# One scores round of batch 2, its keys and its softmax, one position earlier in the first stage

## What is computed

```
B, H, S, D = 8, 8, 576, 64;  pool = 8
k_p, v_p = k, v averaged over groups of 8 keys             # 72 keys
attn = softmax(q @ k_p^T / sqrt(D));  x = attn @ v_p       # 4608 tokens x 512
h = (x @ w1) * (x @ w2) @ w3;  x = h @ w_out               # 512 -> 1024 -> 1024 -> 512
e = argmax(x @ w_gate + modality_bias[modality_id]);  g = softmax(...)[e]
out = g * (relu(x @ w1[e]) @ w2[e])                        # 8 experts, 512 -> 1024 -> 512
```

## Time and profile before

| | |
|---|---|
| Median of 3 runs | 1188.93 us (1187.56 to 1189.38) |
| Profiled execution | 1191.04 us |
| Its span in the trace | 1189.3 us |
| Mean granted clock of PE in it | 0.996 |
| PE busy | 1154.7 us, 97% |
| DVE, ACT, POOL busy | 641.3, 397.3, 404.3 us |

### The profile page before, as it was taken

One profiled execution on the slowest core, in us unless ns is written; L12 is line 12 of the kernel. 1 busy time (PEld: TensorE's weight loads), 2 busy tenths in 40 slices (PEclk: granted clock), 3 DMA queues, 4 the chain that ended last, 5 costly groups with the idle time before them and its releaser, 6 DMA issues.

```text
span 1189.3 us, 29760 instructions
## 1 busy us (share of the span) xinstructions
PE 1154.7 (97%) x12126; PEld 1083.7 (91%) x12127; DVE 641.3 (54%) x1228; ACT 397.3 (33%) x906; POOL 404.3 (34%) x385
## 2 busy tenths in 40 slices
PE   8899989999999999999999999999999999999996
PEld 7678879999999999999999999998998999899895
DVE  0799688898987974753444557622222252222222
ACT  1566455555555541333223224111111141111110
POOL 2355866777766645550000000211211212121111
PEclk9999999999999999999999999999999999999998
DMA  9755362644726414345555555241111101111111
GB/s 349 266 173 149 100 198 78 201 121 148 197 79 200 102 44 125 107 133 140 134 138 135 135 163 176 70 179 45 46 51 35 44 27 55 44 52 45 35 48 41
DMA packets 99890, 137.12 MB, mean 115 GB/s; under 512 B 16835, under 2 KB 66115, under 8 KB 99780
## 3 DMA queue, kind: packets, MB, share of 16 engines
q1 hardware_dynamic: 40340, 78.77, 22.4%
q10 hardware_dynamic: 53040, 36.29, 10.8%
q0 software_dynamic: 6400, 20.50, 5.4%
HBM read 92.99 MB, written 43.06 MB: 114 GB/s over the span
## 4 chain that ended last, share of the span: by engine, by line
PE 55%; DVE 0%; POOL 0%; issue 0%; DMA 0%; ACT 0%; ACTq 0%; POOLq 0%; DVEq 0%
PE ab L728 6%; PE x2p L727 6%; PE ab L727 6%; PE ab L729 6%; PE x2p L729 6%; PE x2p L728 6%; PE rt L728 6%; PE rt L727 6%; PE rt L729 6%; PE sct L916 1%; PE ab L907 0%; DMA out<-y_out,tok_c 0%; DVE gl L1537 0%; POOL gst L635 0%; DVE kb L1511 0%
## 5 line engine op out<-in xcount | busy, mean ns | idle before, releaser
L728 PE MATMUL ab<-xtl,e1h 128*128 128x256 f32 x608 | 170.7, 281 | 0.0
L727 PE MATMUL ab<-xth,e1h 128*128 128x256 f32 x608 | 169.6, 279 | 0.0
L729 PE MATMUL ab<-xth,e1l 128*128 128x256 f32 x608 | 169.3, 278 | 0.0
L1400 ACT ACTIVATE hth<-ab 128x512 fp32r<-128x512 f32 x76 | 45.4, 597 | 333.9 <-PE ab L729 316.7
L707 POOL DMA_INDIRECT out<-y_out,tok_c x38 | 38.4, 1010 | 319.6 <-DVE y_out L2019 319.0
L1998 DVE SCALAR_TENSOR_TENSOR htl<-ab,hth 128x512 fp32r<-128x512 f32 x76 | 52.4, 691 | 156.2 <-ACT hth L1400 151.6
L728 PEld LDWEIGHTS ab<-xtl,e1h 128*128 128x128 f32 x608 | 114.5, 188 | 0.7
L727 PEld LDWEIGHTS ab<-xth,e1h 128*128 128x128 f32 x608 | 114.1, 188 | 1.0 <-issue 0.4
L729 PEld LDWEIGHTS ab<-xth,e1l 128*128 128x128 f32 x608 | 114.3, 188 | 0.0
L1085 ACT ACTIVATE pb<-pb,rc 128x72 f32<-128x72 f32 x320 | 83.2, 347 | 58.9 <-DVE rc L1472 58.9
L727 PE MATMUL ab<-xh,wh 128*128 128x256 f32 x336 | 96.4, 287 | 4.2 <-DVE kb L1511 2.9
(11 more groups left out here) (229 smaller groups left out, 3346.5 us busy)
## 6 DMA issues: line engine op xcount, KB each, us to landing
gr<-g_rows SPq DMA_DIRECT2D x36, 512.0 KB, 4.4
kv<-in_v SPq DMA_DIRECT2D x24, 512.0 KB, 4.9
qt<-in_q ACTq DMA_DIRECT2D x38, 256.0 KB, 3.3
kv<-in_k SPq DMA_DIRECT2D x16, 576.0 KB, 5.4
g_rows<-gst ACTq DMA_DIRECT2D x72, 128.0 KB, 2.8
g_rows<-gst ACTq DMA_DIRECT2D x36, 256.0 KB, 3.3
x_rows<-xr SPq DMA_DIRECT2D x36, 256.0 KB, 4.1
stage<-in_moe_w SPq DMA_DIRECT2D x8, 1024.0 KB, 10.5
```

The lines of the kernel that those rows point to most:

```text
L727: pe.matmul(outp, lh, rh, start=first, stop=False)
L728: pe.matmul(outp, lh, rl, start=False, stop=False)
L729: return pe.matmul(outp, ll, rh, start=False, stop=last)
L1400: act.activation(hth[:, 2 * n:2 * n + 2, :].rearrange("p f n -> p (f n)"), ab[n // 2][:, n % 2, :], ACT.Relu).then_inc(hth_ready, 1)
```

## The change

Round 0 of batch 2 goes on PE from behind product 4 of position 3 to behind product 4 of position 2 of stage 0. Its maximum and subtraction, its sum and inverse (DVE) and its exponential (ACT) go to position 2 as well; its normalising (ACT) goes to the end of position 3, its transpose (DVE) to one place earlier in position 0 of stage 1. POOL pools the keys of batch 2 (both halves) directly behind the second product of position 1 instead of behind the first quarter of position 2. Since the scores now come ahead of the weighing of batch 1, the wait of round 0 for the copied outputs of batch 1 goes, and the weighing waits for the subtraction of round 0 instead, as in the later stages. Nothing is added or taken out.

```diff
--- before.py
+++ after.py
@@ -650,7 +650,7 @@
                     first_quarter(POS * b + i)
                     if i == 0 and b + 1 < B:
                         pool_v(b + 1, 2)
-                    if i == (1 if b else 2) and b + 2 < B:
+                    if b and i == 1 and b + 2 < B:
                         pool_k(b + 2, 0)
                         pool_k(b + 2, 1)
                     if b and i == 2 and b + 2 < B:
@@ -658,6 +658,9 @@
                     if i == 3 and b + 2 < B:
                         pool_v(b + 2, 1)
                     other_quarters(POS * b + i)
+                    if b == 0 and i == 1:
+                        pool_k(2, 0)
+                        pool_k(2, 1)
 
             pool.wait_ge(pv_done, 2 * B)
             pool.memset(ident[:, :], 0.0).then_inc(pool_done, 1)
@@ -790,9 +793,7 @@
                     pe.wait_ge(sub_done, r)
                 if b == 1 and m == 0:
                     pe.wait_ge(xf_ready, 5)
-                if b == 2 and m == 0:
-                    pe.wait_ge(xf_ready, 8 + 5)
-                if b > 2 and m == 0:
+                if b > 1 and m == 0:
                     pe.wait_ge(xf_ready, 8 * (b - 2) + 5)
                 if b and m == 1:
                     pe.wait_ge(xf_ready, 8 * (b - 1) + 5)
@@ -814,7 +815,7 @@
                     pe.wait_ge(vp4_in, 64 * (b + 1))
                     if b == 0:
                         pe.wait_ge(w34_copied, w34_no(FC - 2, 0))
-                    if b > 1 and b + 1 < B:
+                    if b and b + 1 < B:
                         pe.wait_ge(sub_done, AT * (b + 1) + 1)
                 else:
                     pe.wait_ge(xf_ready, 8 * b + 4)
@@ -865,7 +866,7 @@
                         weigh_v(1, 0)
                     if i == 3 and n == 1:
                         weigh_v(1, 1)
-                    if i == 3 and n == 4:
+                    if i == 2 and n == 4:
                         score(2, 0)
 
             def position(b, i):
@@ -1267,6 +1268,7 @@
                     store_g(1, 1)
                     norm(1, 4)
                     store_g(2, 0)
+                    exp_p(2, 0)
                 if i == 3:
                     raw_x(1, 0)
                     copy_p(3, 0)
@@ -1283,7 +1285,7 @@
                 if i == 3:
                     hi_x(1, 4)
                     hi_x(1, 5)
-                    exp_p(2, 0)
+                    norm(2, 0)
 
             def position(b, i):
                 at = POS * b + i
@@ -1295,7 +1297,6 @@
                         exp_p(b + 1, 1)
                     copy_p(at, 1)
                     if b == 1:
-                        norm(2, 0)
                         exp_p(2, 1)
                     store_g(at - 1, 1)
                     if att:
@@ -1730,7 +1731,9 @@
                     u2(2)
                     u3(2)
                     soft_turn(1, 4)
+                    soft_max(2, 0)
                     u4_c22(2)
+                    soft_sum(2, 0)
                 if i == 3:
                     u2(3)
                     x_sum(1, 3)
@@ -1742,7 +1745,6 @@
                     x_sum(1, 5)
                     lo_x(1, 1)
                     lo_x(1, 2)
-                    soft_max(2, 0)
                 c12(i)
                 if i == 3:
                     for n in range(3, 6):
@@ -1760,7 +1762,7 @@
                     u2(at)
                     if b == 1:
                         lo_x(1, 6)
-                        soft_sum(2, 0)
+                        soft_turn(2, 0)
                     u3(at)
                     if b == 1:
                         soft_max(2, 1)
@@ -1768,7 +1770,6 @@
                         soft_max(b + 1, 2)
                     u4_c22(at)
                     if b == 1:
-                        soft_turn(2, 0)
                         soft_sum(2, 1)
                         soft_max(2, 2)
                     if att:
```

## The result

| | before | changed |
|---|---|---|
| Median (22 runs each) | 1187.80 us (1185.84 to 1190.47) | 1190.40 us (1187.66 to 1193.47) |
| Ratio | | 1.0022, 95% interval 1.0015 to 1.0029 |
| Profiled execution, its span | 1191.04, 1189.3 us | 1189.49, 1187.8 us |

The change makes the kernel **slower, by 2.6 us or 0.22%**. I had forecast -0.4 us. The median of 1190.40 us lies inside my range of 1186.6 to 1190.6 us, but by luck: the range was laid round the median of three runs, 1188.93 us, and that of 22 runs is 1187.80. The difference is what failed.

The account below looks back on a forecast made before the run. PE, 97% busy, bounds the kernel, and DVE bounds PE in this stretch. A start 2.50 us later and a run 2.87 us shorter give -0.4 us: 1188.5 us from the 1188.93 median, range 1186.6 to 1190.6.

Parts of the forecast that it names:

- What leaves the run: DVE's gapless run from 131.78 to 156.93 us loses round 0's softmax work, 2.87 us: 22.28 instead of 25.15 us.
- what it costs at the start: PE waits 1.7 us at round 0 for POOL's keys, plus 0.81 us of round: DVE's run starts 2.50 us later.
- The wait for the keys: PE at round 0 of batch 2, near 122.3 us, stands still 1.7 us for the keys pooled by POOL.
- the wait of product 2 of stage 1: PE's wait for DVE there, 1.91 us at 143.50 before, was to fall to about 0.6 us.
- Product 0: First product of stage 1 on PE: at 141.0 instead of 138.5 us, with a wait of over 1 us.
- rival 3: POOL behind position 1: the keys come later still, pooling stretched to 7.85 us; +1.7 us, 1190.6 us; chance 0.07.
- The two x_sums: DVE sums with two SBUF inputs, 1.04 and 1.66 us: waits for POOL shift between them and cancel, taken as 0.
- rival 1: Keys in time at round 0, or DVE pays less to POOL: -2.1 us, 1186.9 us; chance 0.17.
- rival 2: Lock between DVE and POOL falls worse, each x_sum waiting a whole POOL instruction: +0.8 us, 1189.7 us; chance 0.15.
- The signs that I had named for being right: Key wait about 1.7 us; product 2's about 0.6, product 0's over 1; u2 near 134.3 us, round 3 near 156.7.
- The sum: DVE's run ends at 156.56 against 156.93 us, 0.37 us sooner; round 3 and later waits move with it: net -0.4 us.
- SP's loads of values wait for the pooled keys and start some 3 us sooner: Side effect on SP's queue, counted with the other moved work as costing zero.

Follow-up runs that it names:

- loads_wait: Changed kernel with SP's loads of batch 3's keys and spreading of batch 2's values held until round 4's queries landed; 1187.44 us, 0.9999 to the kernel before.
- spread_held: Changed kernel with only the spreading of batch 2's values held until round 4's queries landed; 1188.48 us, 0.9993 to the kernel before.
- before_again: The kernel before, with no edit, profiled a second time; 1188.93 us, ratio 1.0000.

## Why the prediction was wrong, by its own steps

**What held.** *What leaves the run* and *what it costs at the start*: DVE's run in the changed kernel, its first and its last row:

```profile
131.21 0.69 DVE L1512 TENSOR_TENSOR kb<-rt,kb 128x512 f32<-128x512 f32 x1 [6.06 <-PE rt L732]
...
152.61 0.76 DVE L1461 TENSOR_TENSOR pb<-sct,mx 128x576 f32<-128x576 f32 x1
```

It lasts from 131.21 to 153.37, 22.16 us (22.28 forecast). The wait for the keys was 1.73 us (1.7), the wait of product 2 of stage 1 0.40 (0.6). Product 0 waited 0.80, where I had said over 1. The run starts 21.90 us into M instead of 19.18, +2.72 (2.50 forecast), and ends 0.27 us sooner (0.37). The keys themselves came 5.66 us behind the end of POOL's product (113.38 to 119.04), 5.73 by my count; rival 3 was not it. The two x_sums took 1.71 and 1.11 us, 2.82 together against 2.70: they meet POOL's instructions differently and give nearly the same sum, as laid out. Neither rival 1 nor 2 came. The signs that I had named for being right came too, one of them smaller; all of them stand at round 3 or ahead of it, and the loss is behind it.

**The step that failed** is the end of *The sum*: "PE is behind it from there on, and the waits behind 160 us hang on the same order of work, so they move with it." One of them does not. Round 4's start was set by the landing of its queries, which hangs on SP's bulk loads, and these on c12 in the middle of the run, not on its end. The gain at the end of the run stops there, and the delay of 1.14 us at c12 goes through; with a landing 0.5 us slower (12.0 against 11.5 us) this gives the +1.59 us at round 4 (162.98 - 109.31 = 53.67 into M, against 52.08), and the clock the other 0.78. loads_wait shows it from the other side: without the coupling M is 59.30, the change is worth -0.24 us in one profile, and my -0.4 would have stood. The same sentence fails a second time, hidden behind the first: round 0 of batch 3 hangs on POOL's keys, and these on a store that SP's loads hold up, which by the estimate above would have put M at 60.4 alone.

**The sentence with it** is "SP's loads of values wait for the pooled keys and start some 3 us sooner", booked at zero. It is true of the loads of values, but I did not follow SP's queue to the next item, the loads of batch 3's keys and the spreading, and did not ask whose transfers they meet.

**The rivals** lacked this one: a transfer that takes the place of the wait removed. None of the three ended over 0.2% slower; the one called slower put its price on batch 2's keys coming later still, and they came as computed. To a time over 0.2% slower I had given a chance of 0.08.

**What stays open.** The median moved by 2.6 us and M by 2.4, and holding the loads brought 3.4 us in the median and 2.7 in M; the intervals of the ratios (about 1 us to each side) allow both. How much of it the clock has in an average execution is not separated: I have one or two profiles per kernel. What the held-up store costs apart from the query wait is an estimate for the changed kernel; spread_held bears it out in its one profile and not in its median. Nor does a run say why the landing took 11.5 us in one execution and 13.0 in another. After the query waits of 1.9 to 2.45 us the clock fell in all four profiles that have one (0.66 to 0.68 over the 5 us behind the wait). It also fell in kernels without such a wait, at other places.

## What to carry to other kernels

A start that has two reasons at once shows one or none of them as a wait: when a stretch is to be shortened, compare the landing of every transfer and the end of every result needed behind it with the start of its user, and look at the weight loads' waits as well as at PE's. A wait that is found can hide the next: here, behind the late queries stood the late keys. A chain that is shortened behind a branching point moves its end but not what branches off: list the consumers of the middle (here c12, POOL's values, SP's loads) and ask what they collide with. On a crowded stretch, holding the bulk loads back behind the small transfer that is needed next did more than issuing the small one sooner.

## What was not expected of the hardware

- A 256 KB load of queries took 3.3 us in the median of 38 before, but 9.5 us beside 1.9 MB of SP's loads, and 11.9 us when it was issued 0.12 us behind SP's first (151.87 against 151.75) instead of 2.41 us (153.41 against 151.00): it landed 12 us behind the start of SP's loads both times. Held apart from them it took 4.4 us.
- PE's granted clock fell behind waits of about 2 us (0.66 over 5 us), with waits of 1.6 and 1.25 us some 10 us ahead of it. In the first profile of the kernel before, waits of 2.29 and 1.91 us at 152.69 and 157.08 had no such effect, and in its second profile the clock fell at 142 to 146 and at 156 to 160, the second time behind waits of 0.86 and 1.90 us (rounds 2 and 3).
- Where PE waits for DVE anyway, a stretch at the lower clock can take the place of the waits and cost almost nothing: before_again has M = 59.59 with 0.57 granted over 4 us, against 59.54 without, and waits of 0.60 and 0.37 us less.
